# An attention and MLP kernel: a second buffer for split weight sums, other orders of loads and of the end of attention, and row factors that go by way of DRAM

## The reference

```python
# q, k, v: 4 batches x 8 heads x 576 x 64; f: 4 x 8 x 576
scores = (q @ k.T) / 8                                 # per head
cum = cumsum(log(clip(f, 1e-4, 1)))
scores = where(causal, -1e9, scores + cum[:, None] - cum[None, :])
attn = exp(scores - max); attn /= attn.sum + 1e-9
x = (attn @ v)  -> 2304 tokens x 512
xn = x / sqrt(mean(x * x) + 1e-6) * rms_g              # per token
x = (silu(xn @ w_gate) * (xn @ w_val)) @ w_out         # first layer, d_ff 1536
g = x @ w_in
out = (g * sigmoid(g)) @ w_out2                        # second layer, d_ff 2048
```

## Time and profile before

| what | value |
|---|---|
| runs, median (lowest to highest) | 1037.66 us (1034.42 to 1037.98) |
| profiled execution, its own time | 1032.13 us |
| its span | 1030.3 us |
| mean granted TensorE clock | 0.992 |
| attention | from 12 to about 200 us |
| down pieces of g = 0 | from 254.9 us to about 290 us |
| down pieces of g = 1 | until about 375 us |

### The profile page before, as it was taken

How to read it: one execution, slowest core, us unless ns; L and a number is a source line. 1 busy time by engine, 2 the same in 40 slices (tenths; PEclk the granted TensorE clock), 3 DMA queues, 4 the chain that set the end, 5 groups by cost and what they waited for, 6 DMA issues and landing times.

```text
span 1030.3 us, 16304 instructions
## 1 busy us (share of the span) xinstructions
PE 989.9 (96%) x5904; PEld 899.0 (87%) x5904; DVE 646.4 (63%) x1264; ACT 451.7 (44%) x968; POOL 314.0 (30%) x248
## 2 busy tenths in 40 slices
PE   5999999898899879999999999999999999999998
PEld 4777777697799879999999999998989889898996
DVE  5777778477647839778878189751756327562451
ACT  4776687534335314434324235252543326243350
POOL 2665543321311146433524235112030211302112
PEclk9999999999899989999999999999999999999999
DMA  7466545256713656657857757545243544534312
GB/s 240 152 222 186 158 144 172 68 193 248 273 63 150 248 225 235 245 213 279 285 219 255 262 213 249 192 174 194 111 185 134 188 180 163 190 108 182 154 31 92
DMA packets 58591, 192.58 MB, mean 187 GB/s; under 512 B 8272, under 2 KB 19024, under 8 KB 52368
## 3 DMA queue, kind: packets, MB, share of 16 engines
q1 hardware_dynamic: 58512, 191.54, 51.9%
HBM read 150.02 MB, written 41.49 MB: 186 GB/s over the span
## 4 chain that ended last, share of the span: by engine, by line
PE 79%; DVE 7%; DMA 5%; ACT 3%; issue 3%; POOL 2%; SPq 1%; DVEq 0%; ACTq 0%; POOLq 0%
PE banks L1668 15%; PE banks L1670 14%; PE banks L1669 14%; PE banks L1801 6%; PE banks L1800 6%; PE banks L1799 6%; PE banks L1614 4%; PE banks L1582 4%; PE banks L1553 4%; DMA kept<-ws 3%; PE banks L1556 1%; DMA stage_d<-w 1%; DVE scratch L1402 1%; POOL wd L751 1%; DVE ws L1245 1%
## 5 line engine op out<-in xcount | busy, mean ns | idle before, releaser
L1668 PE MATMUL banks<-xb,wu 128*128 128x384 f32 x864 | 289.2, 335 | 5.5 <-DVE x_sb L1170 2.9
L1670 PE MATMUL banks<-xb,wu 128*128 128x384 f32 x864 | 288.7, 334 | 0.0
L1669 PE MATMUL banks<-xb,wu 128*128 128x384 f32 x864 | 288.7, 334 | 0.0
L751 POOL TENSOR_TENSOR wd<-stage_d,wd 128x512 fp32r<-128x512 f32 x84 | 120.0, 1436 | 490.4 <-ACT wd L934 490.4
L1668 PEld LDWEIGHTS banks<-xb,wu 128*128 128x128 f32 x864 | 162.2, 188 | 6.7 <-DVE x_sb L1170 3.0
L1669 PEld LDWEIGHTS banks<-xb,wu 128*128 128x128 f32 x864 | 162.2, 188 | 0.2
L1670 PEld LDWEIGHTS banks<-xb,wu 128*128 128x128 f32 x864 | 162.2, 188 | 0.0
L993 ACT ACTIVATE scratch<-scratch 128x384 f32<-128x384 f32 x144 | 75.4, 523 | 112.9 <-DVE scratch L1360 51.1
L1002 ACT ACTIVATE hid_main<-scratch 128x384 fp32r<-128x384 f32 x144 | 72.2, 517 | 117.1 <-DVE scratch L1402 117.1
L1668 PE MATMUL banks<-hid_main,wd 128*128 128x384 f32 x288 | 100.6, 349 | 19.6 <-POOL wd L751 19.6
L1409 DVE TENSOR_TENSOR hid_main<-scratch,hid_main 128x384 fp32r<-128x384 f32 x144 | 88.3, 627 | 40.6 <-ACT hid_main L1002 36.3
(11 more groups left out here) (163 smaller groups left out, 1698.8 us busy)
## 6 DMA issues: line engine op xcount, KB each, us to landing
wu<-kept SPq DMA_DIRECT2D x48, 1792.0 KB, 10.8
stage_d<-w SPq DMA_DIRECT2D x84, 256.0 KB, 2.8
kept<-ws SPq DMA_DIRECT2D x20, 1024.0 KB, 5.3
qk_raw<-qk_t SPq DMA_DIRECT2D x16, 576.0 KB, 3.5
cum_b<-cum_dram SPq DMA_DIRECT2D x32, 288.0 KB, 5.4
kept<-wu SPq DMA_DIRECT2D x12, 768.0 KB, 4.3
kept<-ws SPq DMA_DIRECT2D x8, 768.0 KB, 5.3
v_sb<-v_p SPq DMA_DIRECT2D x16, 320.0 KB, 4.6
```

The costliest lines, as they stand in the source:

```text
L751: nc.gpsimd.tensor_tensor(wd[:, d % 2, 1, :], stage_d[:, d % 2, :], f32(wd[:, d % 2, 0, :]), ALU.subtract).then_inc(wd_split, 1)
L1668: nc.tensor.matmul(dst, w_hi_part, m_hi, start=start, stop=False)
L1669: nc.tensor.matmul(dst, w_hi_part, m_lo, start=False, stop=False)
L1670: return nc.tensor.matmul(dst, w_lo_part, m_hi, start=False, stop=stop)
```

## The change

Seven things change.

1. Row factors. `row_sum` is now 128 columns wide and zero beyond the nine factors; one transpose (turn entry "r") turns it, ScalarE (VectorE in one pair) copies 9 x 128 to `factors`, and SP stores them in DRAM and loads them back in four broadcasts into `row_scale`. `exps` writes its sums in an order (`sum_at`) that puts the tiles of a head next to each other. `spread`, `rest_scale`, `same_head` and `two_ident` go.
2. `x_out(p - 2, 0)` moves from the end of round p - 1 to the start of round p, ahead of `x_out(p - 2, 1)`.
3. `load_factors(p - 1)` stands at the start of round p of SP's list; the loads of units 2 to 4 stand behind the last of them.
4. Odd units of the first layer have their sums split in a part of `xb` (the place of T3, T1, T4, unused until g = 2) in place of `ws`; each buffer has a semaphore. The rounding of T blocks of the second span waits for the last store out of it.
5. SP in the first layer: of a cycle's sums the first is stored ahead of `load_down(g, 2)` and `(g, 3)`, and the others behind `load_up`; in g = 1 `load_unit(12)` moves behind the down loads; the next unit of the second layer is loaded behind the `raw` slot.
6. The slot ("down", g) of ScalarE and GpSimd stands behind the last down piece for every odd g, not for g = 1 alone.
7. End of attention: the splits of B21, B12 and B22 and the `normalise_x` that they need move forward, `row_factors` of the last pair stands ahead of `values(..., 1, (0, 1))`, and the two waits stand inside cycle 0: for the turn copies ahead of its third product, for x ahead of its last.

```diff
+        def ws_of(q):
+            if q < UNITS1 and q % 2 == 1:
+                return xb[:, 0, 4:7]...[:, 0:2 * SUMS].rearrange("p (b n) -> p b n", b=2)
+            return ws
+            def load_factors(p):
+                turn = TURN[p, "r"]
+                sp.wait_ge(out_act if by_scalar(turn) else out_dve, copies(turn, by_scalar(turn)))
+                sp.dma_start(factors_dram[p:p + 1, :]..., factors[:, :]).then_inc(factors_out, 16)
+                sp.wait_ge(factors_out, 16 * (p + 1))
+                wait(sp, x_done, 2 * p)
+                for hh in range(2):
+                    ...
+                    sp.dma_start(row_scale[hh * DH:(hh + 1) * DH, 0:P * NFULL], full.to_broadcast([DH, P * NFULL]))...
+                    sp.dma_start(row_scale[hh * DH:(hh + 1) * DH, P * NFULL:SEQ], last.to_broadcast([DH, REST]))...
...
+                if p > 0:
+                    load_factors(p - 1)
                 if p + 2 < NPAIRS:
                     load_qk(p + 2)
...
             def x_out(p, part):
                 dve.wait_ge(pv_done, 2 * p + part + 1)
-                wait(dve, out_act, copies(TURN[p, "r0"], True))
-                dve.wait_ge(out_dve, copies(TURN[p, "r1"], False))
+                dve.wait_ge(row_scale_in, 64 * (p + 1))
...
                 if p > 1:
+                    x_out(p - 2, 0)
                     x_out(p - 2, 1)
...
             def row_factors(p):
-                pe.wait_ge(factors_spread, p + 1)
-                turn_free(p, "r0")
-                ...
+                pe.wait_ge(inverted, p + 1)
+                turn_free(p, "r")
+                nc.tensor.transpose(turn_bank(p, "r")[:, 0:P], row_sum[:, p % 2, :], ident[:, :])...
...
             def w_sums(q):
                 act.wait_ge(s_made, 4 * q + 4)
-                wait(act, ws_out, 16 * (ws_outs(q, "sums") - 1))
+                wait(act, ws_sem(q), 16 * (ws_outs(q, "sums") - 1))
...
                 if p == NPAIRS - 1:
                     xb_high(0, "B11")
+                    xb_high(0, "B21")
...
-            pe.wait_ge(x_done, 2 * NPAIRS)
-            pe.wait_ge(out_act, copies(len(TURN) - 1, True))
-            pe.wait_ge(out_dve, copies(len(TURN) - 1, False))
...
                         for c in PLAIN_ORDER:
+                            if n == 0 and c == 3:
+                                pe.wait_ge(out_act, copies(len(TURN) - 1, True))
+                                pe.wait_ge(out_dve, copies(len(TURN) - 1, False))
+                            if n == 0 and c == 1:
+                                pe.wait_ge(x_done, 2 * NPAIRS)
```

176 lines of the change are left out of this document (81 added, 95 removed).

## The result

The changed kernel takes 1027.04 us (median of 7 runs, 1024.24 to 1028.43); the kernel before, on the same chip, 1033.9 us (7 runs, 1032.44 to 1037.98). The ratio is 0.9923, with a 95% interval of 0.990 to 0.9946: faster by 0.8%, not by the 2.9% of the forecast, and 1 us above the forecast range. Of the 29.7 us that the forecast took off its 1037.7, 6.9 came. The profiled execution took 1028.43 us, its span is 1026.5 us and its mean granted clock 0.993.

The account below looks back on a forecast made before the run. TensorE's matmul row, busy 96% of the span, was taken as the bound. Savings 3.4 - 1 + 6.1 + 7.1 + 8.7 + 2.9 = 27.2 us gave 1004.9 from the profiled execution or 1010.5 from the median; forecast 1008, range 998 to 1026.

Parts of the forecast that it names:

- End of attention: Attention's end: TensorE 6.1 us earlier, from waits of 1.79 and 2.90, two row factors and some 0.4 of short waits.
- Order of loads and jobs: First layer: earlier loads save 8.7 us in g = 1, jobs moved behind down splits 2.9 in g = 3 and 5.
- g = 0 and the buffer: First layer, g = 0: without ScalarE's store waits, shorter TensorE waits and no half clock; 7.1 us taken of 13.5.
- Two side effects on SP's queue: Attention: q and k load behind the trip, next store behind the burst's tail (about 0.5 us); 10.75 us a pair.
- R: Start of a pair's row factors on TensorE in attention, from which the forecast counts its times.
- this loop: SP's queue in attention: burst 8.2, store behind its tail 0.5, issues 2.1, together 10.8 us a round.
- X: Attention: when the factors are back from DRAM, put at R+6.5; no gain at all from R+7.6.
- wrong if pairs exceed 11.5 us: The forecast's sign against itself: attention pairs above 11.5 us, where it took 10.75, would show it wrong.
- Rival B: Trip through DRAM paces attention: X near R+7.6 to R+8.5, pair 11.0 to 11.9, 1011 to 1024 us; chance 0.15.
- Rival D: Attention's trip at full-queue prices, store and loads 5.4 us each: pair 16.6, 1090 us, slower; chance 0.09.
- The first means: Attention: the two first means wait for a product that now stands later, costing 1 us.
- The 0.51 us a pair: Attention: TensorE time saved per pair, as one transpose replaces four and the small product.

Follow-up runs that it names:

- both by ScalarE: Changed kernel with the store of the factors and the loads of q and k both issued by ScalarE: 1023.97 us, ratio 0.9908.
- the store alone: Changed kernel with the old row factors, plus in SP's list only a factors store and the wait for its receipt, 14 times, no loads: 1004.09 us, ratio 0.9706.
- the three unread trips: Changed kernel with old row factors, plus an SP trip nothing reads: four full loads 1024.21 us, no loads 1004.09 us, four loads of 32 columns 1022.40 us.

## Why the prediction was wrong

**Outside attention it was right** in the sum, 23.1 us against 24.8, less so in the terms. End of attention: 6.1 forecast, 6.9 measured. Order of loads and jobs (g = 1 and g = 3 and 5): 11.6 forecast, 8.9 measured by the ratios and 3.8 by the traces. The waits of 1.43 came back as said (1.45 and 1.46), the 7.33 did not. Ahead of pieces 3 and 4 of g = 1 TensorE waited 0.97 + 7.33 us before, 4.97 + 0.88 with the old order of loads, 4.97 with the new one, and 1.50 in the changed kernel: the buffer alone took part of it, and the 4.97, a pass of GpSimd, is in no term of the forecast. g = 0 and the buffer: 7.1 forecast, and 11 is what is left over. That the terms' errors nearly cancel is luck in part. No wait of the first layer is above 1.5 us and no stretch at half clock is left from 206 to 400 us, as was said; ScalarE's 23.0 us are gone, but for 3.2 for the last store out of `xb`.

**The step that failed is "Two side effects on SP's queue".** It put the load of q and k at R+8.2 to R+9.1, the cast 0.1 to 0.3 us late, and the next store 0.5 us behind the burst's tail; from these came 10.75 us a pair. Measured in the round at 92 us, whose own receipt is not late: q and k out at R+4.76 (forecast R+4.6), the last small piece issued from R+6.0 (R+5.75), and the cast at R+9.97. The piece lands 4.0 us after its issue begins, where the forecast let it have 2.5 to 3.4; the median of such pieces on the page of the profile went from 3.4 to 3.7. So the cast waits 1.0, not 0.1 to 0.3.

The other half was mis-sized more. The burst was to end some 8 us after its first issue, at R+12.4. Its last issue begins at 100.75, R+8.7, and `cum_t` lands in 5.3 us (median): R+14.0, 9.3 us after its first issue. The next store is out at R+11.9. It does not graze the tail, it has 2.1 us of it ahead, and its receipt of 3.94 us puts the next q and k back, hence the next burst, hence the store after that, unless that round was itself so long that the queue has emptied. That fits rounds of 10.5 and 16 us one behind the other, but it is not all of them: the two rounds with the first means last 15.87 and 15.68 us where the receipts are 1.25 and 1.24 (both by ScalarE), and 12.04 with the store alone. Summed over the 15 receipts, what exceeds 1.22 us is 16.5 us; the casts waited 16.2. They overlap in the same rounds, and how they make the 19 together is not shown.

**That it is the issues** is shown by the three unread trips: store and receipt alone cost nothing, the four loads 16 us (by 0.0156 over the kernel without a trip) at 288 KB and 15.6 at 24 KB. Held against the kernel with the store alone, whose GpSimd pass is the short one as in these two, it is 0.0191 and 0.0186, 19 to 20 us. The rows of the store alone have the arithmetic: from the store of 85.12 to the receipt 1.59 us, to the last issue (90.43, the second of the row at 89.88) 3.7, and `cum_t` lands in 5.1 (median): 10.4 of a round of 10.98. It just closes. With 2.4 us more it is 12.8, and the store stands behind the burst. The forecast did run this loop ("8.2 burst, 0.5, 2.1 of issues: 10.8"), with each term too small. Measured in the round at 92 us: 9.3 from the first issue of q and k to the landing of `cum_t`, 1.29 at the least for a receipt and 2.3 on average over the 15, for which the loop has 0.5 though X has 1.6, and 2.67 from the first of the four issues to q and k. That is 13.3 us where it had 10.8. A round can be shorter, as 11.2 us at 92, only because the next store does not wait for the burst to end, and then its receipt is late. The forecast's own sign, "wrong if pairs exceed 11.5 us", came true with 12.4.

**Rival B** named the right place, the trip in SP's queue, and gave 1011 to 1024, with the row factors as the late thing (X = R+7.6 to R+8.5). Measured in the round at 92 us, `row_scale` had landed by R+7.2. It is late only in rounds with a late receipt. **Rival D's** reason against itself, "a longer pair empties the queue, so the store meets it idle", is right in five of 15 rounds; in the others the receipt took 1.6 to 5.8 us, and the loads landed in 2.7, so its 5.4 for each was too dear. The first means, put at 1 us, had waits of 3.35 and 3.11, a second term that was too small; the run with the means later brought no time, so on that evidence this was a place of waiting and no cause.

**The receipt's price.** The 2.0 us that the prediction takes from the Trainium skill, "DMA: Bandwidth & Descriptors", section "Anatomy of one DMA — SWDGE (gpsimd) path", are given there for a DMA that GpSimd issues. This store goes out on SP, where it took 1.22 us with nothing ahead; from GpSimd it took 1.9 in the two quiet rounds.

**The 0.51 us a pair** that TensorE saves are real (the one transpose costs 0.13 us to the next start, 92.03 to 92.16, and five rounds with a prompt receipt last 10.66 on average against 10.99), but no version of the trip tried here beats the old row factors. What stays open is how late receipts and late casts add up round by round, and what makes the rounds of the first means so long; no sum here gives 12.4 from its parts, and what the lower clock in attention (0.96, where it was 1.00) costs is not separated from them.

The best kernel of the study, leaving aside the one with a store that nothing reads, is the change without its trip: 1006.88 us, ratio 0.9741 (0.9719 to 0.9763), the same ratio with either order of VectorE.
